# Moving the upper four heads' row moves of y from SyncE's queue to ScalarE's, behind ScalarE's copy of y

## The reference

```
for t in range(S):
    cur = einsum('bhd,bhe->bhde', u * k[t], v[t])
    y[:, :, t] = einsum('bhd,bhde->bhe', r[t], state + cur)
    state = w[t][..., None] * state + einsum('bhd,bhe->bhde', k[t], v[t])
x = y.transpose(0, 2, 1, 3).reshape(3072, 384)
h = x @ w_in                              # 384 -> 2048
x = (h * clip(h + 3, 0, 6) / 6) @ w_out   # 2048 -> 384
out = (((x @ w1) * (x @ w2)) @ w3) @ w_out2   # 384 -> 1024 -> 1024 -> 384
```

## Time and profile before

| | |
|---|---|
| time, median of 3 runs | 1024.69 us (1022.93 to 1025.47) |
| profiled execution | 1022.78 us |
| its span, first to last instruction | 1021.0 us |
| PE busy | 945.6 us, 93% |
| DVE busy | 552.5 us, 54% |
| ACT busy | 307.0 us, 30% |
| POOL busy | 244.4 us, 24% |

### The profile page before, as it was taken

One profiled execution on the slowest core, in us unless ns is written; L12 is line 12 of the kernel. 1 busy time (PEld: TensorE's weight loads), 2 busy tenths in 40 slices (PEclk: granted clock), 3 DMA queues, 4 the chain that ended last, 5 costly groups with the idle time before them and its releaser, 6 DMA issues.

```text
span 1021.0 us, 15635 instructions
## 1 busy us (share of the span) xinstructions
PE 945.6 (93%) x6320; PEld 767.9 (75%) x6320; DVE 552.5 (54%) x743; ACT 307.0 (30%) x502; POOL 244.4 (24%) x209
## 2 busy tenths in 40 slices
PE   2579849998999999999999999999999999999997
PEld 1356547777777877877787787787888888888886
DVE  1884558787877677777777853463222222222221
ACT  0113213424333333333323343453213132313222
POOL 0453335344435353535362500000000000000000
PEclk9779959999999999999999999999999999999999
DMA  9953454544342343434334101331101010100000
GB/s 281 298 165 96 131 159 118 138 112 114 110 116 84 112 132 96 133 78 151 90 109 101 55 17 31 120 114 31 63 0 62 1 62 1 62 1 31 1 31 32
DMA packets 79831, 92.84 MB, mean 91 GB/s; under 512 B 9367, under 2 KB 71822, under 8 KB 79630
## 3 DMA queue, kind: packets, MB, share of 16 engines
q1 hardware_dynamic: 69278, 82.13, 28.1%
q10 hardware_dynamic: 10480, 9.70, 3.5%
HBM read 76.07 MB, written 11.01 MB: 85 GB/s over the span
## 4 chain that ended last, share of the span: by engine, by line
PE 77%; DVE 11%; issue 4%; SPq 3%; ACT 2%; DMA 2%; POOL 1%; ACTq 0%; DVEq 0%
PE ps_acc L1008 9%; PE ps_lv L1036 8%; PE ps_h L1008 8%; PE ps_h L1010 8%; PE ps_h L1009 8%; PE ps_acc L1010 8%; PE ps_acc L1009 8%; PE ps_lv L1009 3%; PE ps_lv L1010 3%; PE ps_lv L1008 3%; PE ps_h L1144 3%; DVE k_sb L754 2%; DVE r_sb L754 2%; PE ps_att L1070 2%; DVE totals L754 2%
## 5 line engine op out<-in xcount | busy, mean ns | idle before, releaser
L559 ACT ACTIVATE g_hi<-gated 128x512 fp32r<-128x512 f32 x144 | 90.9, 631 | 395.6 <-DVE gated L902 262.7
L509 POOL TENSOR_TENSOR tok_a<-tok_a 128x384 f32<-128x384 f32 x120 | 144.0, 1227 | 256.0 <-DMA tok_a<-in_k 256.0
L1036 PEld LDWEIGHTS ps_lv<-r_sb,k_sb 48*128 48x128 f32 (+3 forms) x1792 | 94.4, 179 | 59.4 <-issue 46.0
L1036 PE MATMUL ps_lv<-r_sb,k_sb 48*128 48x64 f32 (+3 forms) x1792 | 101.9, 266 | 36.5 <-DVE A_own L824 23.6
L990 DVE TENSOR_TENSOR gated<-gated,ps_lv 128x512 f32<-128x512 f32 x48 | 33.1, 689 | 189.2 <-PE ps_lv L1010 189.2
L910 DVE TENSOR_TENSOR g_lo<-gated,g_hi 128x512 fp32r<-128x512 f32 x96 | 80.0, 833 | 87.5 <-ACT g_hi L559 87.5
L1008 PE MATMUL ps_acc<-g_hi,w_out_hi 128*128 128x512 f32 x288 | 122.2, 424 | 0.0
L1008 PE MATMUL ps_h<-x_hi,w_in_hi 128*128 128x512 f32 x288 | 115.5, 401 | 1.9 <-DVE gated L902 1.8
L1009 PE MATMUL ps_h<-x_hi,w_in_lo 128*128 128x512 f32 x288 | 114.7, 398 | 0.0
L1010 PE MATMUL ps_h<-x_lo,w_in_hi 128*128 128x512 f32 x288 | 114.7, 398 | 0.0
L1009 PE MATMUL ps_acc<-g_hi,w_out_lo 128*128 128x512 f32 x288 | 114.4, 397 | 0.0
(11 more groups left out here) (96 smaller groups left out, 1574.1 us busy)
## 6 DMA issues: line engine op xcount, KB each, us to landing
tok_a<-in_r SPq DMA_DIRECT2D x85, 192.0 KB, 3.0
tok_a<-in_w SPq DMA_DIRECT2D x42, 192.0 KB, 3.7
v_sb<-in_v SPq DMA_DIRECT2D x12, 384.0 KB, 3.6
x_scratch<-x_out SPq DMA_DIRECT2D x6, 768.0 KB, 4.1
x_in<-x_scratch SPq DMA_DIRECT2D x6, 768.0 KB, 6.0
out<-x_out SPq DMA_DIRECT2D x6, 768.0 KB, 3.8
tok_a<-in_k SPq DMA_DIRECT2D x22, 192.0 KB, 4.2
w3T_sb<-in_w3T ACTq DMA_DIRECT2D x8, 512.0 KB, 19.7
```

The lines of the kernel that those rows point to most:

```text
L509: return nc.gpsimd.tensor_tensor(dst, x, y, ALU.mult)
L559: return nc.scalar.activation(dst, src, ACT.Copy, **scale)
L1036: last = nc.tensor.matmul(psum[0:count, h, first:first + C // 2] .rearrange("s (n l) -> s n l", l=size), k_g[rows, cols.start:cols.start + ...
```

## The change

SP issues only the moves of heads 0 to 3 of each chunk. ACT issues those of heads 4 to 7 right behind its copy of y. It first waits for its own copy to be complete (`y_out`), and from chunk 2 on for `x_lo_done` of two chunks before, as SP does.

```diff
             def move_x(g):
                 sp.wait_ge(y_out, g + 1)
                 if g >= 2:
                     sp.wait_ge(x_lo_done, g - 1)
-                for head in range(H):
+                for head in range(H // 2):
...
             def y_copy(g):
                 act.wait_ge(y_done, g + 1)
                 if g >= 2:
                     act.wait_ge(x_moved[g % 2], CHUNK_X * (g // 2))
                 copy(flat(y_sb[g % 2]), ps_att[0:HP, :]).then_inc(y_out, 1)
+                act.wait_ge(y_out, g + 1)
+                if g >= 2:
+                    act.wait_ge(x_lo_done, g - 1)
+                for head in range(H // 2, H):
+                    row, at_row = head * D, head % 2 * HB
+                    while row < (head + 1) * D:
+                        n = min(P - row % P, (head + 1) * D - row)
+                        act.dma_start(x_sb[g % 2][row % P:row % P + n, row // P, :],
+                                      y_sb[g % 2][at_row:at_row + n, head // 2, :]
+                                      ).then_inc(x_moved[g % 2], 16)
+                        row, at_row = row + n, at_row + n
```

## The result

The changed kernel takes 1048.86 us, median of four runs (1046.94 to 1049.86), and the kernel before, on the same chip, 1024.32 us (1022.93 to 1025.47). The ratio is 1.023 (1.0205 to 1.0256). It is slower, as forecast, but by 24.5 us in place of 5.4, and outside the range (1024.5 to 1035).

A forecast was written before the change was run, and what follows sets the result against it. PE was taken as close to full in the loop, so ACT and SP changes matter only where PE waits. Losing 6.9 us in the loop and gaining 1.5 in the ramp made 5.4 us longer: 1030.0 us, range 1024.5 to 1035.

The forecast's parts named there:

- The price of an issue on ACT: Five moves issued on ACT at SP's price, 5 x 0.62 = 3.1 us, bounds 2.5 and 4.2 us.
- READ_A covers them: At READ_A, ACT's issues fall in idle time (7.40 us in group 4), so they cost nothing.
- READ_B does not: At READ_B, ACT's issues delay g_hi, g_lo and DVE's totals by 0 to 2.0 us a group; 6.9 us lost.
- the ramp: End of the ramp, chunk 3: moves land 3.1 us earlier, 1.6 lost beside POOL, 1.5 us gained (bounds 0 and 3.1).
- the forecast 29 us of waits for the merge: PE's waits for DVE's masked merge, 23.6 us before, were to become 23.6 - 1.5 + 7, some 29 us.
- In the loop nothing waits for that: In the loop, SP's five saved issues (3.1 us a chunk) gain nothing; its next loads are wanted many us later.
- the list of what would make it wrong: ACT's issues much shorter, totals started by PE's signal in all groups, or POOL's earlier products changing DVE's durations beyond the delays.
- the sum for the loop: Six READ_B delays reaching PE in full through DVE: 6.9 us lost in the loop.
- one rival: Issues cheaper, or delays absorbed as POOL's products fall beside other DVE operations: 1024.9 to 1026.5 us; chance 0.29.
- the clock had a place only in the ramp: Only the faster rival counted PE's clock: a shorter gap at the ramp's end might give back some 1.5 us.
- The rival of dearer issues: SP's simultaneous tok loads lengthen ACT's issues at READ_B by 1.1 us each: 1038 us, or 1033 if milder; chance 0.10.
- the faster rival: The ramp's whole 3.1 us reach PE and the loop costs nothing: 1021.6 us, 1020 with the clock; chance 0.08.

The follow-up runs named there:

- The fillers: Ten unread matmuls of 384 columns per group from group 3, ahead of products awaiting the first merge: changed kernel 1037.39 us, kernel before 1029.48 us.

## Why the prediction was right in direction and wrong in size

**Right, and nearly to the row.** The price of an issue on ACT (0.61 us against 0.62, five in 3.1); that READ_A covers them (the run with even chunks alone loses nothing); that READ_B does not, and that g_hi, g_lo and the totals are late by what was worked out (0.73 us in group 4 for 0.7, and in the kernel with SP's queue kept full 2.0, 1.5 and 1.6 in groups 2, 3 and 6 for 2.0, 1.4 and 1.5); the ramp (1.7 for 1.5), with POOL beside k_sb and r_sb. The kernel that has these things and no other (SP's queue kept full) has the forecast 29 us of waits for the merge, though even it lost 11.4 us in all, some 4 of them in PE's clock. In the changed kernel itself the totals of groups 2 and 6 were 3.5 and 2.4 us late, since g_lo too ran beside POOL there, and in group 2 the issues took 3.7 us.

**Wrong: "In the loop nothing waits for that".** The prediction priced SP's five saved issues at nothing because the next loads are wanted many us later. That is so for PE, but the one that waits for a load is POOL: in the changed kernel it waits 281.7 us for its tiles (before: 256.0), and whenever a tile comes earlier, POOL starts earlier. In group 4 it began 1.2 us earlier after the copy of y, the hold moved DVE's totals 0.7 us later, and the two met. The first scaling took 30.9 us in place of 15.4 over eight groups. The text priced just this in the ramp (two operations, 0.8 us each) and, in the list of what would make it wrong, named POOL's earlier products, but the sum for the loop had no term for it, and one rival took them for a help to DVE. The Trainium skill (page SBUF — State Buffer, section Who interferes with whom) says that a DVE instruction with two SBUF inputs contends with a GpSimd instruction that reads SBUF, and that the order of issue decides who is blocked. The trace agrees on which operations suffer: totals go from 0.29 to 1.10 us and k_sb from 0.68 to 1.50, and the merge, with its data in PSUM, takes 1.23 beside POOL.

**Wrong: the clock had a place only in the ramp.** Every delay in the loop was counted at its own length in PE's waits. In fact the sum of the waits grew by 10.0 us and PE's busy time by 16.4, since behind the longer waits PE worked 3 to 10 us at 1.2 GHz, in eight stretches where the kernel before had one. The fillers showed this term by itself.

**So the sum would have been**: waits 10.0 (forecast: 5.4, ramp included) and busy time 16.4 (forecast: nothing), together 26.4 between the two profiled executions. The rival of dearer issues would have come nearer in time, but for a cause that did not happen: only three of nine batches were dearer, by 0.3 to 0.6 us. The time of the faster rival (1020 to 1021.6) came in a version that was not the change, the one with no hold at READ_B, at 1020.3 us; that this is the ramp's gain and nothing else is not shown.

## What to carry to other kernels

When an edit makes an engine late, look in the timeline for what the late work then runs beside, and do the same for each engine that the edit makes earlier: here delays of 0 to 2 us in a group were forecast at about 5 us in all and cost 24.5, because they moved DVE's three operations into POOL's, and the shorter queue of SP moved POOL's towards them. Where the bound is PE, a wait that is added to a full loop is to be priced with what the clock takes afterwards (here 16 us beside 10 us of waits). DMA issues on a compute engine cost nothing in these runs where they fitted into idle time, and the same five made 28.6 us of difference by one slot.

## What was not expected of the hardware

*Short waits and the clock.* That waits of 1 to 2 us are followed by some 3 us at half clock was not expected, and not every such wait is. Windows of the kernel before and then of the changed kernel, in group 3:

```profile
234.00:238.00 4.00, 4.00 (x37) 3.49 (x36) 3.14 (x5) 1.55 (x3) 2.23 (x2) 1.00 0.35 114
238.00:242.00 4.00, 4.00 (x41) 3.29 (x40) 3.30 (x4) 1.23 (x3) 4.00 (x5) 1.00 0.48 152
```

```profile
238.00:242.00 4.00, 4.00 (x21) 3.27 (x19) 2.10 (x3) 1.62 (x3) 2.93 (x3) 0.59 0.58 173
```

In both, PE had waited 0.86 and then 1.01 us in the 8 us ahead of this, for the same instructions (at 230.08 and 233.45; at 233.30 and 236.67). The clock stayed at 1.00 in the one and fell to half in the other. What decides between them stays open.

*Two issuing engines and the landing.* With SP and ACT issuing at once a move took 2.6 us from issue to landing at the median, where it took 1.8 with SP alone. It cost nothing here: in the loop x is wanted later, and at the end of the ramp, where x_hi waits for the moves, it starts 1.24 us behind the end of SP's last issue in both kernels (136.40 to 137.64 before, 132.88 to 134.12 now).
